# Tile 0's attention in two halves of the keys, joined by token rows

## The chip, the cores and the metric

One NeuronCore of a Trainium2 chip runs the whole program: TensorE (PE in the rows), VectorE (DVE), ScalarE (ACT), GpSimd (POOL) and the DMA queue of SyncE (SP). The metric is the device time of one execution in microseconds, the median over several runs. Lower is better.

## The reference, cut to what matters

Three steps follow each other on 12288 tokens of 128 channels: attention of q to 768 keys that are pooled from kv, and two FFNs with 2048 hidden columns.

```python
kv_pool = kv.reshape(B, H // 4, 4, W // 4, 4, C).mean(axis=(2, 4))   # 384 x 32 pixels -> 96 x 8 = 768 keys
k = v = kv_pool.reshape(B, -1, C) @ w_sr
s = (q @ k.transpose(0, 2, 1)) / np.sqrt(C)
a = np.exp(s - s.max(-1, keepdims=True))
a /= a.sum(-1, keepdims=True) + 1e-09
x = (a @ v)                                      # [12288, 128]
h = x @ w_in;   x = (h * sigmoid(1.702 * h)) @ w_out          # first FFN
h = x @ w_in2;  y = (h * clip(h + 3, 0, 6) / 6) @ w_out2      # second FFN
```

## The kernel before, in words

The tokens are cut into 24 tiles of 512. A tile has 4 slots of 128 tokens. Every fp32 product is made of three fp32r matmuls: each operand is split into a high part, copied by ScalarE (or POOL for the weights), and a low part, subtracted by VectorE (or POOL), and `product` (L799 to L802) issues high by high, high by low and low by high. Each engine has its own list of instructions, written out by hand, which it works off strictly in order; semaphores join them.

**kv and keys.** SyncE loads kv in 8 groups of 768 KB (pixels of 4 columns of the image), the last one in three rows of 256 KB, then the q tiles 0 and 1, then the four weight matrices (1 MB each), then q of tile 2. For each group VectorE adds two pairs of pixels (`add_pixels`, L566), and TensorE pools it to 96 keys with 6 matmuls against `patch` (`pool_group`, L814; a matmul of plain fp32 shows as two records). ScalarE copies the pooled part out, TensorE multiplies it by w_sr (`keys_of`, L821), ScalarE and VectorE split it into k_hi and k_lo. The values are the keys transposed by TensorE (`values_of`, L827). Keys go in parts of 384, 288 and 96; the two halves of the keys (384 each) lie in the two banks of a pair of PSUM banks.

**Tile 0 before.** Its scores (`scores`, L830 on) take all 768 keys per slot and begin once the keys' last part is split. VectorE takes the maximum (L610), ScalarE the exponential with the row sum (L406), TensorE turns the probabilities by chunks of 128 keys (`turn_probs`, L852), ScalarE and VectorE split them (L411, L632), TensorE weighs the values (`weigh_first`) into bank_av, which holds channels by tokens. 1/sum goes through DRAM to reach all partitions (`spread_inv`), and `scale_x` (L648) multiplies it in. Tile 1's scores and exponentials are slipped between these steps. `x1_high` and `x1_low` (L652) split x, ScalarE loads the table for gelu (L470), and the first FFN of tile 0 begins: `hidden1(0, p)` and `project1(0, p - 2)` for p = 0 to 7, with gelu (L438), act1_hi (L445) and act1_lo (L660) between them. The probabilities of tile 1 are transposed by VectorE (`turn_p`, L627) among these.

**Weights.** POOL splits them in 16 pieces of 512 columns (L356, L359) as they land. `hidden1(0, p)` waits for piece p // 2, `project1(0, p)` for piece 4 + p // 2, and `hidden2(0, 0)` for all of them.

**From tile 1 on** TensorE alternates jobs of the first FFN of tile i and the second FFN of tile i - 1; `between(i)` scores tile i + 2 and weighs the values of tile i + 1. This part is a loop on all engines.

Of the kernel before, what the change touches and what calls it, by code (L numbers as in the profile page):

```python
# [5 lines left out]
ALU = mybir.AluOpType  # L6
ACT = mybir.ActivationFunctionType
F32 = mybir.dt.float32
# [4 lines left out]
def attention_and_two_ffns(nc, q, kv, w_sr, w_in1, w_out1, w_in2, w_out2, out):  # L13
# [7 lines left out]
    HALF = KEYS // 2  # L21
    SLOTS = 4
# [4 lines left out]
    N_KV = KV_GROUPS * KV_ROWS * R  # L27
    GROUP_KEYS = HH // R
# [15 lines left out]
    q_rows = q.rearrange("b (n i) c -> i (b n) c", i=32)  # L44
    out_rows = out.rearrange("(n i) c -> i n c", i=32)
# [4 lines left out]
    with ExitStack() as ctx:  # L50
# [38 lines left out]
        v_hi = sb("v_hi", [128, KEYS], F32R)  # L89
        v_lo = sb("v_lo", [128, KEYS], F32R)  # L90
# [4 lines left out]
        y_sb = sb("y_sb", [128, TILE])  # L95
        w_sr_sb = sb("w_sr_sb", [128, C])
# [6 lines left out]
        p_sum_eps = sb("p_sum_eps", [128, SLOTS])  # L103
        p_inv = sb("p_inv", [128, 32])
# [5 lines left out]
        probs_first = work[:, 2 * PAIR:2 * PAIR + SLOTS * KEYS]  # L110

        pooled = p_keys[:, 0:KEYS]
        k_full = p_keys[:, KEYS:2 * KEYS]
        q_raw1, q_t1 = y_sb, x_full
        q1_hi, q1_lo = x2_hi, x2_lo

        def mid2(t, p):
# [3 lines left out]
        pair = [psum(f"pair{n}", 2 * 512) for n in range(3)]  # L121
        bank_av = psum("bank_av", 512)
        bank_out = psum("bank_out", 512)

        PART_AT = [0, HALF, KEYS - GROUP_KEYS, KEYS]
        PART_GROUPS = [KV_GROUPS // 2, KV_GROUPS - 1, KV_GROUPS]
        PART_POOL = [pair[0][:, 0:HALF], pair[0][:, 512:512 + HALF - GROUP_KEYS], bank_av[:, 0:GROUP_KEYS]]
        PART_KEYS = [pair[1][:, 0:HALF], pair[1][:, 512:512 + HALF - GROUP_KEYS],
                     bank_av[:, 128:128 + GROUP_KEYS]]
        PARTS = 3  # L130
# [7 lines left out]
        def scores_in(u, s):  # L138
            if isinstance(u, int) and u == 0:
                return pair[(0, 1, 2, 0)[s]]  # L140
            if isinstance(u, int) and u == 1:
                return pair[(1, 0, 1, 0)[s]]
            return pair[(0, 2, 1, 0)[s]]
# [8 lines left out]
        def hidden1_in(t, p):  # L152
            return pair[0] if isinstance(t, int) and t == 0 and p % 2 else pair[2]
# [16 lines left out]
        kv_row_loaded = [sem(f"kv_row_loaded{a}") for a in range(KV_ROWS)]  # L170
        q_loaded = sem("q_loaded")
        q1_loaded = sem("q1_loaded")
# [6 lines left out]
        kv_added = sem("kv_added")  # L179
# [3 lines left out]
        k_full_ready = sem("k_full_ready")  # L183
# [5 lines left out]
        qt_ready = sem("qt_ready")  # L189
# [896 lines left out]
```

## Time and profile before

| | us |
|---|---|
| median of 3 timed runs (1304.80 to 1305.52) | 1305.46 |
| the profiled execution's own time | 1302.91 |
| its span | 1301.2 |
| TensorE busy | 1275.8 (98%) |
| VectorE, ScalarE busy | 1038.3 (80%), 1031.9 (79%) |
| GpSimd busy | 38.0 (3%) |
| 16 DMA engines, queue of SyncE | 22.4% of their span |

A row of the timeline gives the start in us from the span's start, the duration (for several equal instructions in a row: from the first's start to the last's end), engine, line, operation, tiles and shapes, the count, and in brackets how long the engine had been idle and what released it. The duration of a matmul holds its way through the array; matmuls that follow each other start closer than that. The granted clock (PEclk) is a share of 2.4 GHz.

### The profile page before, as it was taken

The numbers are of one execution on the slowest core, as the hardware profiler recorded it, in microseconds if no ns is written. First come the engines' busy times: TensorE is split into PE (matmuls) and PEld (weight loads), VectorE is DVE, ScalarE is ACT, GpSimd is POOL, SyncE is SP. The second block draws the span as 40 slices with busy tenths as digits, with TensorE's granted clock in tenths as the row PEclk, the third lists the DMA queues.
The fourth block names the chain that finished last, engine by engine and source line by source line (L and its number), as shares of the span: only waits on it lengthen the run. The fifth ranks groups of instructions, "written<-read, shape, count | busy, mean of one in ns | idle before, by whom it ended". The sixth has DMA issues, their size and how long they took to land.

```text
span 1301.2 us, 18295 instructions
## 1 busy us (share of the span) xinstructions
PE 1275.8 (98%) x5748; PEld 1061.1 (82%) x5748; DVE 1038.3 (80%) x1072; ACT 1031.9 (79%) x1211; POOL 38.0 (3%) x43
## 2 busy tenths in 40 slices
PE   6899999999999999999999999999999999999998
PEld 5678888888888888888888888888888888888786
DVE  4788888878888888888788888887888888877667
ACT  2688888788888887888888878888788788887776
POOL 0910000000000000000000000000000000000000
PEclk9999999999999999999999999999999999999999
DMA  8331303213023032130230321302303213022001
GB/s 268 107 71 44 69 5 73 48 24 73 23 50 71 1 73 48 24 73 22 51 71 2 73 48 24 73 21 51 71 2 73 48 24 73 21 44 65 1 9 17
DMA packets 186884, 65.94 MB, mean 51 GB/s; under 512 B 108656, under 2 KB 179440, under 8 KB 186608
## 3 DMA queue, kind: packets, MB, share of 16 engines
q1 hardware_dynamic: 185808, 65.56, 22.4%
q10 hardware_dynamic: 1056, 0.13, 0.1%
q8 instruction: 10, 0.16, 0.1%
q14 instruction: 10, 0.08, 0.0%
HBM read 23.13 MB, written 6.34 MB: 23 GB/s over the span
## 4 chain that ended last, share of the span: by engine, by line
PE 96%; DVE 2%; ACT 1%; DMA 1%; issue 0%; SPq 0%; ACTq 0%
PE pair L800 16%; PE pair L802 16%; PE pair L801 16%; PE bank_av L800 9%; PE bank_av L802 9%; PE bank_av L801 9%; PE bank_out L802 6%; PE bank_out L801 6%; PE bank_out L800 6%; PE pair L814 1%; DMA kv_sb<-in_kv_dram 1%; DVE neg_max L610 0%; ACT probs L406 0%; DVE p_low L632 0%; DVE mid_lo L660 0%
## 5 line engine op out<-in xcount | busy, mean ns | idle before, releaser
L676 DVE TENSOR_TENSOR mid_lo<-work,mid_hi 128x1024 fp32r<-128x1024 f32 (+1 forms) x193 | 234.9, 1218 | 135.3 <-ACT mid_hi L466 135.1
L800 PE MATMUL pair<-x_hi,w_hi 128*128 128x512 f32 x768 | 301.9, 393 | 4.5 <-DVE x_lo L652 3.3
L801 PE MATMUL pair<-x_lo,w_hi 128*128 128x512 f32 x768 | 299.2, 390 | 0.0
L802 PE MATMUL pair<-x_hi,w_lo 128*128 128x512 f32 x768 | 299.0, 389 | 0.0
L438 ACT ACTIVATE work<-pair 128x1024 f32<-128x1024 f32 x192 | 197.1, 1027 | 125.0 <-PE pair L802 122.6
L660 DVE TENSOR_TENSOR mid_lo<-work,mid_hi 128x1024 fp32r<-128x1024 f32 x192 | 235.3, 1226 | 29.9 <-ACT mid_hi L445 29.9
L669 DVE SCALAR_TENSOR_TENSOR work<-work,pair 128x1024 f32<-128x1024 f32 (+1 forms) x193 | 232.3, 1204 | 4.0 <-ACT work L453 3.6
L453 ACT ACTIVATE work<-pair,half 128x1024 f32<-128x1024 f32 (+1 forms) x193 | 212.2, 1100 | 4.9 <-PE pair L802 4.9
L445 ACT ACTIVATE mid_hi<-work 128x1024 fp32r<-128x1024 f32 x192 | 202.6, 1055 | 5.1 <-PE bank_av L802 2.7
L466 ACT ACTIVATE mid_hi<-work 128x1024 fp32r<-128x1024 f32 (+1 forms) x193 | 201.4, 1044 | 1.9 <-DVE work L669 1.8
L800 PEld LDWEIGHTS pair<-x_hi,w_hi 128*128 128x128 f32 x768 | 144.1, 188 | 43.0 <-ACT work L438 7.0
L802 PEld LDWEIGHTS pair<-x_hi,w_lo 128*128 128x128 f32 x768 | 144.2, 188 | 30.5
L801 PEld LDWEIGHTS pair<-x_lo,w_hi 128*128 128x128 f32 x768 | 144.2, 188 | 28.3
L800 PE MATMUL bank_av<-mid_hi,w_hi 128*128 128x512 f32 x400 | 157.1, 393 | 1.9 <-DVE mid_lo L660 1.5
L802 PE MATMUL bank_av<-mid_hi,w_lo 128*128 128x512 f32 x400 | 155.8, 389 | 0.0
L801 PE MATMUL bank_av<-mid_lo,w_hi 128*128 128x512 f32 x400 | 155.8, 389 | 0.0
L801 PE MATMUL bank_out<-mid_lo,w_hi 128*128 128x512 f32 x368 | 143.2, 389 | 0.0
L800 PE MATMUL bank_out<-mid_hi,w_hi 128*128 128x512 f32 x368 | 143.2, 389 | 0.0
L802 PE MATMUL bank_out<-mid_hi,w_lo 128*128 128x512 f32 x368 | 143.1, 389 | 0.0
L406 ACT ACTIVATE probs<-pair,neg_max 128x768 f32<-128x768 f32 x92 | 82.5, 901 | 72.2 <-DVE neg_max L610 71.2
L610 DVE TENSOR_REDUCE neg_max<-pair 128x1 f32<-128x768 f32 x96 | 89.5, 952 | 19.9 <-PE pair L802 18.8
L800 PEld LDWEIGHTS bank_av<-mid_hi,w_hi 128*128 128x128 f32 x400 | 75.1, 188 | 23.2 <-DVE mid_lo L660 5.9
(88 smaller groups left out, 1506.9 us busy)
## 6 DMA issues: line engine op xcount, KB each, us to landing
p_keys<-p_turned SPq DMA_DIRECT2D x368, 96.0 KB, 2.2
inv_b<-inv_dram SPq DMA_DIRECT2D x24, 256.0 KB, 3.3
out_dram<-y_sb SPq DMA_DIRECT2D x94, 64.0 KB, 2.4
q_raw<-in_q_dram SPq DMA_DIRECT2D x92, 64.0 KB, 2.0
kv_sb<-in_kv_dram SPq DMA_DIRECT2D x7, 768.0 KB, 10.9
w_raw<-in_moe_w_in_dram SPq DMA_DIRECT2D x2, 1024.0 KB, 8.0
inv_dram<-inv_t SPq DMA_DIRECT2D x96, 0.5 KB
kv_sb<-in_kv_dram SPq DMA_DIRECT2D x3, 256.0 KB, 11.7
```

The costliest lines, as they stand in the source:

```text
L406: act.activation(two(slot(dst, s)), halves(scores_in(u, s)), ACT.Exp, bias=neg_max[:, s:s + 1], accum_out=p_sum[:, s:s + 1]).then_inc(exp_ ...
L438: act.activation(act1[p % 2], hidden1_in(t, p)[:, :], ACT.Gelu_apprx_sigmoid).then_inc(act1_ready, 1)
L445: act.activation(mid_hi[p % 2][:, :], act1[p % 2], ACT.Copy).then_inc(mid1_hi_ready, 1)
L453: act.activation(gate2[p % 2][:, part], hidden2_in(t, p)[:, part], ACT.Relu, bias=half[:, :], scale=1.0 / 6.0).then_inc(gate2_ready, 1)
L466: act.activation(mid_hi[mid2(t, p)][:, part], act2[p % 2][:, part], ACT.Copy).then_inc(mid2_hi_ready, 1)
L610: dve.reduce_max(neg_max[:, s:s + 1], halves(scores_in(u, s)), AX_XY, negate=True).then_inc(max_ready, 1)
L660: dve.tensor_tensor(mid_lo[p % 2][:, :], act1[p % 2], mid_hi[p % 2][:, :], ALU.subtract).then_inc(mid1_ready, 1)
L669: dve.scalar_tensor_tensor(out=act2[p % 2][:, part], in0=gate2[p % 2][:, part], scalar=1.0, in1=hidden2_in(t, p)[:, part], op0=ALU.min, op ...
L676: dve.tensor_tensor(mid_lo[mid2(t, p)][:, part], act2[p % 2][:, part], mid_hi[mid2(t, p)][:, part], ALU.subtract).then_inc(mid2_ready, 1)
L800: pe.matmul(dst, a_hi, b_hi, start=start, stop=False)
L801: pe.matmul(dst, a_hi, b_lo, start=False, stop=False)
L802: return pe.matmul(dst, a_lo, b_hi, start=False, stop=stop)
```

## The change

- kv: groups 3, 6 and 7 are loaded by rows. w_sr and q of tile 0 (token rows, 512 B each) stand behind group 1, q of tile 1 behind the last row of kv. POOL does the adds of groups 4 and 5. Keys go in parts of 288, 96, 288, 96.
- q of tiles 0 and 1 is turned by TensorE instead of VectorE. POOL splits q of tile 1, ahead of the weights.
- The values are pooled kv times w_sr, computed again in the other orientation, and v_hi and v_lo lie side by side in `v_cat`.
- Tile 0 is scored against the first 384 keys as soon as these are there, with a maximum, exponentials, a sum and an output of its own; the same follows for the second 384 keys with the maximum of both. The first half is scaled by exp(new maximum - old one) and the two are joined. The output is tokens by channels (`weigh_first`: probabilities stand, 256 columns of v_cat move), so 1/sum is a number per partition and does not go through DRAM. x is turned by TensorE.
- Tile 1's scores: slots 0 and 1 around the turning of x, slots 2 and 3 behind `hidden1(0, 0)`; its four exponentials stand behind `x1_high_first`, and the table load for gelu behind them. VectorE's four `turn_p(1, s)` and `inverse(1)` stand ahead of `act1_lo(0, 0)`.
- From tile 2 on the instructions are the same.

The lists of TensorE, ScalarE and VectorE, and the new steps that the prediction speaks of:

```diff
 # SyncE
+                if g == 1:
+                    sp.dma_start(w_sr_sb[:, :], w_sr).then_inc(w_sr_loaded, 16)
+                    sp.dma_start(q_raw[:, :].rearrange("p (s c) -> p s c", s=SLOTS), q_first).then_inc(q0_loaded, 16)
 # POOL
+            for g in POOL_GROUPS:
+                hold(kv_loaded[g], 16)
+                pool.tensor_tensor(rows[:, :, 0:2 * C], rows[:, :, 0:2 * C], rows[:, :, 2 * C:4 * C],
+                                   ALU.add).then_inc(kv_added[g], 1)
+            hold(q1_copied, 1)
+            pool.tensor_scalar(q1_hi[:, :], q_t[:, :], 1.0, 1.0, ALU.mult, ALU.mult).then_inc(q_hi_ready, 1)
+            hold(q_hi_ready, 2)
+            pool.tensor_tensor(q1_lo[:, :], q_t[:, :], q1_hi[:, :], ALU.subtract).then_inc(q_lo_ready, 1)
             for piece in range(W_PIECES):
 # VectorE, new steps
+            def maximum_first(h, s):
+                dve.wait_ge((a_scores_ready, scores_ready)[h], s + 1)
+                ...
+                dve.reduce_max(neg_max_b[:, s:s + 1], in_chunks(first_in(s)), AX_XY, negate=True).then_inc(b_max_ready, 1)
+                dve.wait_ge(a_max_ready, s + 1)
+                dve.wait_ge(b_max_ready, s + 1)
+                dve.tensor_tensor(neg_max[:, s:s + 1], neg_max_a[:, s:s + 1], neg_max_b[:, s:s + 1],
+                                  ALU.min).then_inc(max_ready, 1)
+            def join_first(s):
+                ...
+                dve.scalar_tensor_tensor(out=x_full[:, cols], in0=first_output(1, s)[:, 0:128],
+                                         scalar=scale_b[:, s:s + 1], in1=a_scaled[:, cols],
+                                         op0=ALU.mult, op1=ALU.add).then_inc(b_high_added, 1)
+                dve.wait_ge(b_high_added, s + 1)
+                dve.scalar_tensor_tensor(out=x_full[:, cols], in0=first_output(1, s)[:, 128:256], ...)
 # VectorE, its list up to the FFN
+            for g in range(KV_GROUPS // 2 - 1):
                 add_pixels(g)
+                if g == 1:
+                    q_low_first()
+            for a in range(KV_ROWS):
+                add_row_pixels(KV_GROUPS // 2 - 1, a)
             k_lo_part(0)
+            k_lo_part(1)
+            for s in range(SLOTS):
+                maximum_first(0, s)
+            v_lo_part(0)
+            p_lo_first(0, 0)
+            ...                        # row adds of groups 6 and 7, p_lo_first(0, 1..3) between them
+            k_lo_part(2); k_lo_part(3)
             for s in range(SLOTS):
+                maximum_first(1, s)
+            shift_first(); v_lo_part(1); p_lo_first(1, 0); scales_first(); a_add_low(0)
+            for s in range(1, SLOTS):
+                p_lo_first(1, s)
+            a_add_low(1)
+            for s in range(SLOTS):
+                join_first(s)
+            for h in range(2):
+                x1_low_first(h)
+            for s in range(SLOTS - 1):
+                maximum(1, s)
+            turn_p(1, 0)
+            maximum(1, SLOTS - 1)
+            for s in range(1, SLOTS):
+                turn_p(1, s)
             inverse(1)
 # ScalarE, the second half of its list
+            k_hi_copy(3)
+            q1_copy()
+            exponential_first(1, 0)
+            exponential_first(1, 1)
+            v_hi_copy(1)
+            exponential_first(1, 2)
+            p_hi_first(1, 0)
+            exponential_first(1, 3)
+            fade_first()
+            a_high_copy(0)
+            p_hi_first(1, 1); p_hi_first(1, 2); p_hi_first(1, 3)
+            a_high_copy(1)
             for s in range(SLOTS):
+                a_scale(s)
+            for h in range(2):
+                x1_high_first(h)
+            for s in range(SLOTS):
+                exponential(1, s)
             load_table(ACT.Gelu_apprx_sigmoid)
 # TensorE
+            pool_group(0); pool_group(1); turn_q_first(0); pool_group(2); pool_loaded_row(3, 0)
             pe.wait_ge(w_sr_loaded, 16)
             keys_of(0)
+            pool_loaded_row(3, 1); pool_loaded_row(3, 2); keys_of(1)
+            pe.wait_ge(k_lo_ready, 2)
+            pe.wait_ge(q_lo_ready, 1)
+            for s in range(SLOTS):
+                scores_first(0, s)
+            values_of(0); pool_group(4); turn_probs(0, 0); turn_probs(0, 1)
+            pool_group(5); turn_probs(0, 2); turn_probs(0, 3)
+            pool_loaded_row(6, 0); pool_loaded_row(6, 1); weigh_first(0, 0)
+            pool_loaded_row(6, 2); weigh_first(0, 1); pool_loaded_row(7, 0)
+            keys_of(2); pool_loaded_row(7, 1); pool_loaded_row(7, 2)
+            turn_q_first(1); keys_of(3)
             pe.wait_ge(k_lo_ready, PARTS)
+            for s in range(SLOTS):
+                scores_first(1, s)
+            values_of(1); turn_probs(1, 0); weigh_first(0, 2); turn_probs(1, 1); weigh_first(0, 3)
+            turn_probs(1, 2); pe.wait_ge(q1_copied, 1); weigh_first(1, 0); turn_probs(1, 3)
+            for s in range(1, SLOTS):
+                weigh_first(1, s)
+            pe.wait_ge(a_summed, 1)
             scores(1, 0)
+            turn_first(0); turn_first(1)
             scores(1, 1)
+            hidden1(0, 0)
+            pe.wait_ge(a_summed, 2)
+            scores(1, 2)
+            pe.wait_ge(exp_ready, SLOTS + 1)
+            scores(1, 3)
+            for p in range(1, PAIRS):
                 hidden1(0, p)
```

(Calls that stand one to a line in the code are put side by side here.)

## Rows read from the trace of the kernel before

**Rows 1.** The page, chain of waits that ended last, by engine.
```profile
PE 96%; DVE 2%; ACT 1%; DMA 1%; issue 0%; SPq 0%; ACTq 0%
```
**Rows 2.** Windows, 48 to 51 us: busy us by engine, then clock, DMA.
```profile
48.00:51.00 3.00, 0.21 (x2) 0.05 (x1) 2.64 (x6) 2.97 (x5) 2.82 (x4) 1.00 0.00 0
```
**Rows 3.** Timeline of ScalarE, 25 to 53 us.
```profile
25.05 0.25 ACT L366 ACTIVATE p_keys<-bank_av 128x96 f32<-128x96 f32 x1 [0.93 <-PE bank_av L814]
25.20 0.62 ACT L397 ACTIVATE q_hi<-q_t 128x512 fp32r<-128x512 f32 x1
...
32.35 0.90 ACT L406 ACTIVATE work<-pair,neg_max 128x768 f32<-128x768 f32 x1
...
49.57 1.28 ACT L470 ACT_TABLE_LOAD   x1
...
52.66 1.03 ACT L438 ACTIVATE work<-pair 128x1024 f32<-128x1024 f32 x1 [1.59 <-PE pair L802]
```
**Rows 4.** Timeline of TensorE, 19 to 60 us.
```profile
19.34 1.52 PE L814 MATMUL pair<-patch,kv_sb 128*128 128x96 f32 x12
...
34.39 0.34 PE L801 MATMUL pair<-k_lo,x_hi 128*128 128x384 f32 x1
34.56 0.35 PE L802 MATMUL pair<-k_hi,x_lo 128*128 128x384 f32 x1
...
35.94 1.97 PE L852 MATMUL pair<-ident,work 128*128 128x128 f32 x8 [0.49 <-ACT work L406]
...
39.34 0.60 PE L852 MATMUL pair<-ident,work 128*128 128x128 f32 x4
...
53.84 0.45 PE L800 MATMUL pair<-x_hi,w_hi 128*128 128x512 f32 x1
...
56.09 0.50 PE L800 MATMUL bank_av<-mid_hi,w_hi 128*128 128x512 f32 x1 [0.65 <-DVE mid_lo L660]
...
59.13 0.50 PE L800 MATMUL bank_av<-mid_hi,w_hi 128*128 128x512 f32 x1
```
**Rows 5.** Timeline of VectorE, the adds of kv groups and of the last row.
```profile
12.20 0.96 DVE L566 TENSOR_TENSOR kv_sb<-kv_sb 128x768 f32<-128x768 f32 x1 [1.05 <-DMA kv_sb<-in_kv_dram]
...
18.26 0.96 DVE L566 TENSOR_TENSOR kv_sb<-kv_sb 128x768 f32<-128x768 f32 x1 [1.07 <-DMA kv_sb<-in_kv_dram]
...
23.43 0.42 DVE L573 TENSOR_TENSOR kv_sb<-kv_sb 128x256 f32<-128x256 f32 x1 [0.26 <-DMA kv_sb<-in_kv_dram]
```
**Rows 6.** Windows of 1 us, TensorE alone: busy, instructions, clock, DMA share, GB/s.
```profile
12.00:13.00 1.00, 1.00 (x6) 1.00 1.02 385
...
16.00:17.00 1.00, 1.00 (x11) 1.00 1.05 385
...
36.00:37.00 1.00, 1.00 (x5) 0.50 0.95 309
```
**Rows 7.** Timeline of VectorE, 25 to 59 us.
```profile
25.85 0.69 DVE L605 SCALAR_TENSOR_TENSOR q_lo<-q_t,q_hi 128x512 fp32r<-128x512 f32 x1 [0.91 <-ACT q_hi L397]
...
27.00 0.25 DVE L580 TENSOR_TENSOR k_lo<-bank_av,k_hi 128x96 fp32r<-128x96 f32 x1
...
35.48 0.96 DVE L610 TENSOR_REDUCE neg_max<-pair 128x1 f32<-128x768 f32 x1 [0.62 <-PE pair L802]
36.36 0.18 DVE L615 TENSOR_SCALAR p_sum_eps<-p_sum 128x4 f32<-128x4 f32 x1
...
50.82 1.82 DVE L627 STREAM_TRANSPOSE p_turned<-probs 128x768 f32<-128x768 f32 x2
54.81 1.23 DVE L660 TENSOR_TENSOR mid_lo<-work,mid_hi 128x1024 fp32r<-128x1024 f32 x1 [2.17 <-ACT mid_hi L445]
...
56.84 2.23 DVE L660 TENSOR_TENSOR mid_lo<-work,mid_hi 128x1024 fp32r<-128x1024 f32 x1
```
**Rows 8.** Timeline of POOL, the first piece of the weights.
```profile
31.37 0.63 POOL L356 TENSOR_SCALAR w_hi<-w_raw 128x512 fp32r<-128x512 f32 x1 [28.73 <-DMA w_raw<-in_moe_w_in_dram]
32.18 1.27 POOL L359 TENSOR_TENSOR w_lo<-w_raw,w_hi 128x512 fp32r<-128x512 f32 x1 [0.18 <-POOL w_hi L356]
```

More of the change, by code:

```diff
@@ L109, in attention_and_two_ffns @@
         act2 = [work[:, n * PAIR:(n + 1) * PAIR] for n in (4, 5)]
[L110 to L114, printed above, removed]
+        probs_half = [work[:, at * PAIR:at * PAIR + SLOTS * HALF] for at in (4, 2)]
+        pooled = probs[:, 0:KEYS]
+        a_scaled = inv_b
+        q_raw1 = y_sb
         q1_hi, q1_lo = x2_hi, x2_lo
@@ L843, in scores, with scores_first @@
                 scores_half(u, s, 1).then_inc(scores_ready, 1)
-            def turn_probs(k):
-                if k > 1:
-                    pe.wait_ge(pt_lo_ready, k - 1)
-                else:
-                    pe.wait_ge(exp_ready, SLOTS)
-                for s in range(SLOTS):
-                    at = (k % 2) * 512 + s * 128
-                    last = pe.transpose(pair[2][:, at:at + 128],
-                                        slot(probs_first, s)[:, k * 128:(k + 1) * 128], ident[:, :])
+            def scores_first(h, s):
+                tok, keys = slice(s * 128, (s + 1) * 128), slice(h * HALF, (h + 1) * HALF)
+                if h == 1:
+                    pe.wait_ge(pt_lo_ready, s + 1)
+                product(first_in(s), q_hi[:, tok], q_lo[:, tok], k_hi[:, keys], k_lo[:, keys], True,
+                        True).then_inc((a_scores_ready, scores_ready)[h], 1)
@@ L867, in weigh, with turn_first @@
+            def turn_first(n):
+                pe.wait_ge(first_x_ready, 2 * (n + 1))
+                for c in range(2):
+                    at = (2 * n + c) * 128
+                    last = pe.transpose(X_FIRST_IN[n][:, c * 128:(c + 1) * 128], x_full[:, at:at + 128], ident[:, :])
+                last.then_inc(xt_ready, 1)
             def weigh(t, k):
@@ L887, in _ @@
+            weigh_first(0, 1)
+            pool_loaded_row(7, 0)
             keys_of(2)
-            pe.wait_ge(k_lo_ready, 1)
-            pe.wait_ge(q_lo_ready, 1)
-            scores_half(0, 0, 0)
-            scores_half(0, 1, 0)
+            pool_loaded_row(7, 1)
+            pool_loaded_row(7, 2)
+            turn_q_first(1)
+            keys_of(3)
             pe.wait_ge(k_lo_ready, PARTS)
-            scores_half(0, 0, 1).then_inc(scores_ready, 1)
+            for s in range(SLOTS):
+                scores_first(1, s)
```

509 lines of the change are left out of this document (312 added, 197 removed).

## The prediction, made before the changed kernel ran

> **What bounds the kernel now.** I read the chain of waits on the page first: TensorE holds 96% of what ended last [rows 1]. So from the second tile on, time is TensorE time, and nothing there is edited: the loop body keeps its instructions. A change to tile 0 can only move the moment at which the dense stretch begins; whatever it moves is kept to the end. Then I read windows of the first 90 us: the last large gap of TensorE ahead of tile 0's FFN is at 48 to 51 us, where it is busy for 0.21 of 3 us [rows 2]. So the event to forecast is the first gelu of tile 0: now at 52.66 us [rows 3], with the third pair of hidden matmuls at 53.84 and the first projection at 56.09 [rows 4]. Its difference is the difference of the kernels, as long as the FFN of tile 0 behind it keeps its pace.
>
> **First half, up to its scores.** VectorE adds a kv group when it lands; groups come 2.03 us apart (12.20 to 18.26 is three of them), the last row is added at 23.43 [rows 5]. Two loads (320 KB; 768 KB take 2.03 us) now stand behind group 1, so the later groups land some 0.9 us later; kv0 and kv1 land some 0.4 us earlier, w_sr no longer being ahead. By landing alone the first half's keys could be pooled at 16 us. But the queues are in order: TensorE pools group 1 (10.8 to 12.7, by 6 matmuls a microsecond, where a later one holds 11 [rows 6]), turns q with four transposes (half of eight in 1.97, 1.0 [rows 4]), ScalarE copies 0.6 [rows 3], VectorE's q_low_first takes 0.7 [rows 7] and ends at 15.1, and only behind it stand the adds of group 2 and of three rows (0.9 + 3 x 0.4). Then on TensorE: group 2 until 17.7, one row 0.5, copy 0.4, keys_of(0) 0.6, two rows 0.9, copy 0.25, keys_of(1) 0.4, k_hi and k_lo 0.25 each [rows 3, 7]. Call the start of scores_first(0, 0) A: **A = 21.3** (bounds 19.3, with TensorE at full rate and no gaps, and 23.5).
>
> **First half, from A to the second half's scores (S).** Prices: a pooling group 1.36 (12 matmuls in 1.52 with the tail of the last, 0.113 apart), a row a third of it, 0.45; a half score 3 x 0.175 = 0.52; transposes 0.088 apart (four in 0.60 with a tail of 0.25), so three 0.26 [rows 4]. weigh_first is 6 matmuls of 256 columns, a width that the trace lacks: between 0.113 (the pooling matmul, 96 columns in two passes) and 0.175 (384 columns); I take 0.122, by the line through 0.2275 at 512 and 0.175 at 384 columns, so 0.73 in all (0.68 to 1.05). TensorE's list is then: four half scores 2.1, values 0.7, groups 4 and 5 2.7, twelve transposes 1.0, rows of group 6 1.4, two weigh_first 1.5, rows of group 7 1.4, keys_of(2) 0.5, turn_q_first(1) 0.35. With the tail copy, keys_of(3), k_hi, k_lo (0.25 each with hand-overs, 1.0) it is 12.7. I walked the other engines beside it: exponential 0.58 (half of the 0.90 [rows 3] and its accumulator read), p_hi and p_lo of 384 0.5 each (between 0.25 for 96 and 0.69 for 512 [rows 7]), and they wait for TensorE more than it for them; the one tight place is pooled_copy(2) ahead of p_hi_first(0, 3) on ScalarE, which holds p_lo and the last row add until A + 10.7, just when TensorE asks for it. So **S = A + 12.7 = 34.0**. At present the same point is at 27.3 (k_lo of the last 96 keys) [rows 7]. The last kv row has then been in SBUF for about 9 us: TensorE, not the load, sets the end of this stage. POOL's adds of groups 4 and 5 (1.9 each by 1.27 for 512 elements, rows 8; at most 4) end by 21 to 25, TensorE wants group 5 at A + 4.7 = 26: covered.
>
> **Second half, from S to the FFN.** VectorE is the limit. Per slot a 384 maximum 0.5 and a one-column minimum behind its own wait 0.2 (half of 0.96, and 0.18 [rows 7]): the four maxima are out at S + 3.65. Then shift 0.2, v_lo 0.55, p_lo 0.55 (S + 5.1), four small ops behind ScalarE's fade 0.85 (S + 6.15), a_add_low 0.35, three p_lo 1.5, a_add_low 0.4 (S + 8.4), eight joins of 128 columns at 0.29 (S + 10.8). TensorE's weigh_first(1, 3) ends at S + 9.3, inside that. Turning by TensorE, x1_hi and x1_lo by halves: S + 12.0; **hidden1(0, 0) at S + 12.1 = 46.1**, where it is at 50.95 now: 4.8 us earlier. What goes with this is the trip of 1/sum through DRAM, which is no loss to anyone now (it had landed long before x_full).
>
> **But the gelu does not follow.** Before, tile 1's exponentials had been slipped between tile 0's steps and the table load lay under the wait for x1_lo. Now all four stand behind x1_high_first on ScalarE, and tile 1's slots 2 and 3 are scored behind hidden1(0, 0). From S + 12.1: hidden1(0, 0) 1.4, scores(1, 2) 1.05, scores(1, 3) 1.05 beside maximum(1, 2), then turn_p(1, 0) in VectorE's order ahead of maximum(1, 3): 15.65 + 0.9 + 0.95 = 17.5 (two turns take 1.82 [rows 7]). Exponential 1.0, table load 1.3, warm 0.25 [rows 3]: gelu at **S + 20.1 = 54.1, 1.4 us later than now**. hidden1(0, 2) waits for it until 55.2 and TensorE has nothing from 51.1 to 55.2: that gap of 4.1 us takes the place of the 2.8 us one. turn_p(1, 1..3) and inverse (3 x 0.9 + 0.6) end at S + 20.8, before act1_lo(0, 0) is due at S + 22.2: free; if they were not, each 0.9 would be added.
>
> **Behind it.** turn_p no longer interrupts act1_lo; the first projections were 3.04 apart (56.09 to 59.13) against 12 x 0.2275 = 2.73 of TensorE work [rows 4], so about -0.3. POOL waits for q1_copied and splits w from about 36.7 instead of 31.4 [rows 8]; the last piece then ends near 76 instead of 70.5, needed at about 85 by hidden2(0, 0): free. But while POOL runs, a VectorE subtract of 1024 takes up to 2.23 instead of 1.23 [rows 7], for 5 us longer: +0.3 (0 to 1).
>
> **The clock.** After 32.2 to 34.1 idle and half an us more the granted clock fell to 0.50, that is 1.2 GHz, for about 3 us, and eight transposes took 1.97 [rows 4, 6]; after the gap at 48 it stayed at 2.4 GHz [rows 2]. The new gap is longer than both. If it falls, hidden1(0, 2) costs 2.8 instead of 1.4 and project1(0, 0) begins under it: worth 1.3 by walking the first four jobs at double price until 60 us; bounds 0 and 3.3. At the front, TensorE's matmuls are slow until about 14.7 now (6 in a microsecond against 11 [rows 6]); with the added gap from 13.7 to 16 some slow rate reaches beyond A: +0.4 (0 to 2).
> The Trainium skill (TensorE: Matmul & The Clock Gate, "Why this matters for your kernels") says to leave no longer idle gaps between bursts, since the clock is halved behind them. By that rule the 1.3 us are due here; without it the sum below is 1.3 us less. It speaks against this change, and the row of 36 to 37 us agrees with it.
>
> **Sum.** +1.4 - 0.3 + 0.3 + 0.8 x 1.3 + 0.4 = about +2.8 us, with 0.8 my weight for the drop of the clock. The profiled execution's own time is 1302.91 (span 1301.2 and 1.7 around it); the timed median is 1305.46, 2.5 above it. I carry the difference over: 1305.46 + 2.6 = **1308.1 us**.
>
> **Rivals.**
> 1. The clock stays up in the new gap, and at the front: +1.4 or less, 1306.8. For it: the gap at 48 us left it alone. Against it: this one is longer, and little runs just ahead of it.
> 2. Faster. The front is set by landing and not by the order of queues: TensorE reaches the full rate before it turns q, A = 19.3 or less, and pooling overlaps so that S is near 30.5. The VectorE chain from S on has 2 us of waiting in it; with none of it gelu is at S + 18.2 = 48.7: -4.0, and 1301.6. It decides from S below 30.0 with the waits, or 31.9 without. For it: kv has landed by 23.3, and hidden1(0, 0) has 4.8 us in hand. Against it: the adds behind q_low_first, and a TensorE list of 12.7 us that is mostly price and not waiting.
> 3. Worse than forecast: scores of the first half run at 1.2 GHz, since TensorE has gaps ahead of them. The list from A gains 2 to 3 us and everything moves: +5.5 to +7, 1311.5. For it: the slow stretch at the start [rows 6]. In this case one would say that the change does not do what it says, half a tile being done "while kv loads" only on paper.
>
> **Chances.** Forecast 0.42 (own range 1306.5 to 1310.5), rival 1 0.22, rival 2 0.20, rival 3 0.16. What the measurement can tell from no change is 0.2%, 2.6 us. Faster than that is most of rival 2: 0.18. Slower is rival 3 and two thirds of the forecast: 0.44. Same: 0.38. Range 1302.0 to 1312.5: up to near rival 2, and all of rival 3 but its tail.
>
> **What would show it.** In the new trace: scores_first(0, 0) near 21.3, the last pooling matmul near 32 with kv in since 23, scores_first(1, 0) near 34, hidden1(0, 0) near 46, the gelu table load near 52.6, gelu near 54, a gap of about 4 us in TensorE before hidden1(0, 2) and a granted clock of 0.5 behind it. Wrong is the forecast if S comes before 31, if weigh_first costs over 1 us, if the exponentials of tile 1 do not hold the table load, or if the dense stretch behind tile 1's start is longer or shorter than now by over 1 us.

## The result: slower by 9.4 us, with the profile after

The kernel after takes 1314.88 us (median of 4 runs, 1314.50 to 1315.92); the kernel before, on the same chip, 1305.49 (4 runs, 1304.80 to 1306.17). By the medians that is +9.4 us (0.72%); the recorded ratio of the two kernels is a little higher, 1.0083, 95% interval 1.0071 to 1.0096. The forecast was 1308.1 (+2.6), its range ended at 1312.5: the sign was right, the size was missed by 6.8 us. The profiled execution's own time is 1315.92, its span 1314.2 (before 1302.91 and 1301.2).

Start with the chain of waits of the kernel after, by engine, beside [rows 1]:

```profile
PE 96%; DVE 2%; ACT 1%; DMA 1%; issue 0%; SPq 0%; DVEq 0%; ACTq 0%
```

Nothing new bounds the kernel. The dense stretch only starts later, and by how much is read at three places of TensorE's timeline: scores_first(0, 0), whose start the forecast calls A, scores_first(1, 0), whose start it calls S, and the first FFN, with the gap in it.

```profile
11.37 2.88 PE L996 MATMUL pair<-patch,kv_sb 128*128 128x96 f32 x12 [1.62 <-DVE kv_sb L694]
14.04 1.06 PE L1031 MATMUL bank_out<-ident,q_raw 128*128 128x128 f32 x4
17.38 2.87 PE L996 MATMUL pair<-patch,kv_sb 128*128 128x96 f32 x12 [2.28 <-DVE kv_sb L694]
20.05 1.06 PE L996 MATMUL bank_av<-patch,kv_sb 128*128 128x96 f32 x4
20.90 1.25 PE L1013 MATMUL pair<-probs,w_sr_sb 128*128 128x288 f32 x2
21.94 1.67 PE L996 MATMUL bank_av<-patch,kv_sb 128*128 128x96 f32 x8
...
25.05 0.45 PE L987 MATMUL pair<-k_hi,q_hi 128*128 128x384 f32 x1 [0.64 <-DVE k_lo L707]
25.34 0.34 PE L988 MATMUL pair<-k_lo,q_hi 128*128 128x384 f32 x1
25.51 0.33 PE L989 MATMUL pair<-k_hi,q_lo 128*128 128x384 f32 x1
...
38.04 0.45 PE L987 MATMUL pair<-k_hi,q_hi 128*128 128x384 f32 x1 [0.64 <-DVE k_lo L707]
...
45.66 0.36 PE L1076 MATMUL pair<-v_cat,p_high 128*128 128x256 f32 x1 [1.77 <-DVE p_low L804]
...
49.61 0.55 PE L1076 MATMUL pair<-v_cat,p_high 128*128 128x256 f32 x1 [2.67 <-DVE p_low L804]
49.96 0.41 PE L1077 MATMUL pair<-v_cat,p_low 128*128 128x256 f32 x1
50.17 0.41 PE L1076 MATMUL pair<-v_cat,p_high 128*128 128x256 f32 x1
...
56.90 0.50 PE L987 MATMUL pair<-x_hi,w_hi 128*128 128x512 f32 x1
...
65.94 0.77 PE L987 MATMUL pair<-x_hi,w_hi 128*128 128x512 f32 x1 [3.89 <-ACT work L548]
...
102.45 0.50 PE L987 MATMUL pair<-x_hi,w_hi 128*128 128x512 f32 x1 [1.11 <-ACT work L548]
```

A is 25.05 and S is 38.04. The rows from 20.05 to 21.94 are the three loaded rows of group 3 with keys_of(0) between them; TensorE did not wait ahead of any of them. hidden1(0, 0) is at 56.90, where it was at 50.95 before. The last row is the third pair of hidden matmuls of tile 1's FFN, the first place that looks alike in both kernels (idle 1.11 us, released by the gelu). It is called the landmark from here on; it stood at 89.42 in the kernel before. Its +13.0 us is the +13.0 us of the spans, so nothing behind it differs. (From the landmark to the end the profiles of all kernels here take 1211.8 to 1212.7 us, so a landmark tells a span to within 0.9 us.) Two waits on VectorE (1.77 and 2.67 us) stand in the middle, and behind the second the matmuls of 256 columns start 0.21 us apart (49.96, 50.17), where they start 0.12 apart elsewhere.

ScalarE's timeline answers to [rows 3]: the table load behind tile 1's last exponential, and the gelu 12.1 us later than before (64.79 against 52.66).

```profile
62.38 0.90 ACT L485 ACTIVATE probs<-pair,neg_max 128x768 f32<-128x768 f32 x1 [0.73 <-DVE neg_max L732]
...
63.38 1.28 ACT L580 ACT_TABLE_LOAD   x1
...
64.79 1.01 ACT L548 ACTIVATE work<-pair 128x1024 f32<-128x1024 f32 x1
```

Now VectorE's timeline. The first two rows are the front; then come the small operations between the maxima and the joins, and last a row of the FFN.

```profile
15.77 0.69 DVE L717 SCALAR_TENSOR_TENSOR q_lo<-bank_out,q_hi 128x512 fp32r<-128x512 f32 x1 [4.46 <-ACT q_hi L467]
...
17.24 2.71 DVE L701 TENSOR_TENSOR kv_sb<-kv_sb 128x256 f32<-128x256 f32 x3
...
39.54 0.96 DVE L744 TENSOR_TENSOR neg_max<-neg_max_a,neg_max_b 128x1 f32<-128x1 f32 x1
...
43.31 1.27 DVE L749 TENSOR_TENSOR shift<-neg_max,neg_max_a 128x4 f32<-128x4 f32 x1
...
45.44 1.19 DVE L754 TENSOR_TENSOR faded_sum<-fade,p_sum_a 128x4 f32<-128x4 f32 x1
46.67 0.54 DVE L757 SCALAR_TENSOR_TENSOR p_sum_eps<-faded_sum,p_sum 128x4 f32<-128x4 f32 x1
47.24 0.18 DVE L760 RECIPROCAL scale_b<-p_sum_eps 128x4 f32<-128x4 f32 x1
47.45 1.21 DVE L762 TENSOR_TENSOR scale_a<-fade,scale_b 128x4 f32<-128x4 f32 x1
...
65.12 0.18 DVE L790 RECIPROCAL p_inv<-p_sum_eps 128x4 f32<-128x4 f32 x1
```

The same operation on four elements takes 0.16 or 1.2 us. Put POOL's timeline beside it:

```profile
17.57 4.05 POOL L434 TENSOR_TENSOR kv_sb<-kv_sb 128x768 f32<-128x768 f32 x2 [14.94 <-DMA kv_sb<-in_kv_dram]
...
39.19 1.29 POOL L439 TENSOR_TENSOR x_lo<-q_t,x_hi 128x512 fp32r<-128x512 f32 x1 [0.18 <-POOL x_hi L437]
...
43.30 1.27 POOL L447 TENSOR_TENSOR w_lo<-w_raw,w_hi 128x512 fp32r<-128x512 f32 x1 [0.18 <-POOL w_hi L444]
...
45.33 1.28 POOL L447 TENSOR_TENSOR w_lo<-w_raw,w_hi 128x512 fp32r<-128x512 f32 x1 [0.18 <-POOL w_hi L444]
46.58 0.62 POOL L444 TENSOR_SCALAR w_hi<-w_raw 128x512 fp32r<-128x512 f32 x1
47.38 1.26 POOL L447 TENSOR_TENSOR w_lo<-w_raw,w_hi 128x512 fp32r<-128x512 f32 x1 [0.18 <-POOL w_hi L444]
...
65.03 0.61 POOL L444 TENSOR_SCALAR w_hi<-w_raw 128x512 fp32r<-128x512 f32 x1
...
69.21 2.07 POOL L447 TENSOR_TENSOR w_lo<-w_raw,w_hi 128x512 fp32r<-128x512 f32 x1 [0.19 <-POOL w_hi L444]
```

Add start and duration: the shift ends at 44.58, POOL's subtract at 44.57; faded_sum at 46.63 and 46.61; p_sum_eps at 47.21 and 47.20; scale_a at 48.66 and 48.64; the first minimum at 40.50 and 40.48. A small operation with two SBUF inputs that begins beside an instruction of POOL ends with it. The reciprocal at 47.24, with one input, falls into a pause of POOL (47.20 to 47.38) and tells nothing; the one at 65.12 runs inside POOL's w_hi (65.03 to 65.64) and still takes 0.18. It also goes the other way: POOL's subtract of 69.21, begun while VectorE's mid_lo was running (68.92 to 70.15), takes 2.07 us instead of 1.28, and VectorE's loses nothing. Taken against 0.16 each, the six that were held (the third minimum, 0.74, is not shown) cost 4.9 us, on the engine that sets the end of this stage.

The windows of TensorE alone (length, busy us with count, granted clock, DMA share, GB/s) show what its gaps bring on:

```profile
48.00:52.00 4.00, 2.39 (x11) 0.50 0.00 0
52.00:56.00 4.00, 3.69 (x21) 0.75 0.02 6
...
64.00:68.00 4.00, 2.06 (x5) 0.53 0.26 62
68.00:72.00 4.00, 4.00 (x12) 0.62 0.66 152
```

From 48 to about 54 us, and again from 66 to 71, TensorE works at 1.2 GHz.

### The profile page after: what moved, and what is told of

It reads as the page before. It is cut to its first block, busy times and chain, and to the rows that moved or that the text cites. A ratio compares the mean times of both kernels' runs of the same rounds, so it can differ in the third digit from the quotient of the medians.

```text
span 1314.2 us, 18413 instructions
## 1 busy us (share of the span) xinstructions
PE 1284.0 (98%) x5798; PEld 1071.1 (81%) x5798; DVE 1042.4 (79%) x1094; ACT 1034.9 (79%) x1228; POOL 40.5 (3%) x47
## 4 chain that ended last, share of the span: by engine, by line
PE 96%; DVE 2%; ACT 1%; DMA 1%; issue 0%; SPq 0%; DVEq 0%; ACTq 0%
PE pair L987 16%; PE pair L989 16%; PE pair L988 16%; PE bank_av L987 9%; PE bank_av L988 9%; PE bank_av L989 9%; PE bank_out L989 6%; PE bank_out L988 6%; PE bank_out L987 6%; PE pair L996 1%; DMA kv_sb<-in_kv_dram 1%; PE bank_av L996 0%; PE pair L1076 0%; PE pair L1077 0%; ACT work L563 0%
## 5 line engine op out<-in xcount | busy, mean ns | idle before, releaser
L732 DVE TENSOR_REDUCE neg_max<-pair 128x1 f32<-128x768 f32 x91 | 84.7, 953 | 18.0 <-PE pair L989 16.9
```

Source lines behind the costliest of these rows:

```text
L732: dve.reduce_max(neg_max[:, s:s + 1], halves(scores_in(u, s)), AX_XY, negate=True).then_inc(max_ready, 1)
```

## Theories

**Theory.** Four things make up the +12.1 us at the gelu, where +1.4 was forecast: A comes 3.75 us late, and three causes are put up for it (VectorE does q_low_first ahead of the adds of group 2, POOL's adds hold up the row adds, TensorE stays slow); S is 0.3 us late besides; from S to hidden1(0, 0) POOL's weight pieces hold VectorE's small operations (4.9 us), and the gap this makes in TensorE costs 1.8 us of clock (18 matmuls 0.21 instead of 0.12 us apart, and the scores behind them).

**Rivals.** The small operations are slow by themselves, behind their semaphores, whoever runs beside them. The front is set by the landing of kv. The 3.9 us gap ahead of hidden1(0, 2), and not the front, is what the change costs.

All experiments start from the kernel after, unless said otherwise. Each ratio is against the kernel before on the same chip: its median was 1304.49 us for experiments 1, 2, 4 and 5, 1304.99 for experiments 3, 6, 7 and 8, and 1306.11 for experiments 9 to 11. The kernel after was timed in its 4 runs only, on yet another occasion (before: 1305.49), so a difference to 1314.88 can be off by about 1 us. Counted against the kernel before on their own chip, the losses are 6.8 us (experiment 1), 7.1 (2), 8.9 (4), 9.5 (5) and 9.7 (6), against the 9.4 of the kernel after: the times show a gain for experiments 1 and 2, and for 5 and 6 none.

## Experiment 1: POOL starts the weights later

```diff
+            hold(scale_a_ready, 1)
             for piece in range(W_PIECES):
```

> Change: the changed kernel, but POOL begins to split the weights only when VectorE's small operations for the joining of the halves are done (it holds on scale_a_ready). Theory 1 (POOL in the way): those of VectorE's operations that read two operands from SBUF wait for POOL's tensor_tensor; then the minimum, shift, faded_sum, p_sum_eps and scale_a, now 0.54 to 1.27 us, fall to about 0.2, the stretch from the second half's scores to hidden1(0, 0) falls from 18.9 to 12.5 to 14 us, TensorE's gap of 2.7 us ahead of weigh_first(1, 1) shrinks and with it the halved clock there; the time falls by 5 to 6.5 us to about 1309. Splitting later costs nothing, since the last piece is then ready near 80 us and needed near 90. Rival: the small operations are slow by themselves, by their waits on one another; then nothing moves (within 1 us), or the time rises because hidden1(0, 0) waits for its weights. The minima beside POOL's split of q of tile 1 stay slow in both theories, 0.8 us.

Measured: 1311.32 us (6 runs, 1310.09 to 1314.74), ratio 1.0053 [1.0039, 1.0068]; 3.6 us less than the kernel after. VectorE's timeline:

```profile
39.50 0.96 DVE L745 TENSOR_TENSOR neg_max<-neg_max_a,neg_max_b 128x1 f32<-128x1 f32 x1
...
42.70 0.16 DVE L750 TENSOR_TENSOR shift<-neg_max,neg_max_a 128x4 f32<-128x4 f32 x1
...
43.92 0.16 DVE L755 TENSOR_TENSOR faded_sum<-fade,p_sum_a 128x4 f32<-128x4 f32 x1
...
44.52 0.16 DVE L763 TENSOR_TENSOR scale_a<-fade,scale_b 128x4 f32<-128x4 f32 x1
...
81.31 5.41 DVE L811 TENSOR_TENSOR p_low<-p_keys,p_high 128x1024 fp32r<-128x1024 f32 x3
```

With POOL silent the same operations take 0.16 us, and the one that still meets POOL (it splits q of tile 1 at 39.2) takes 0.96: the rival of slow small operations falls. S is the same (38.01), hidden1(0, 0) is at 51.12, S + 13.1 instead of S + 18.9, and the gap at 47 to 49.6 us is gone and with it the clock's fall (granted 1.00 there). That is 5.8 us; of these, 4.1 are the small operations, and the rest, 1.6 by the spacing of the 18 matmuls, the clock. Both went with one edit, so the clock's part is read off and not tested by itself. The last row shows where part of it goes again: POOL now splits weights until 88 us, and three subtracts of 1024 take 5.41 us instead of 3.49; TensorE waits 1.13 us at 87.37 for the x_lo that stands behind them. At the landmark -4.7 is left (97.79).

## Experiment 2: the front in another order

```diff
 # POOL, ahead of the adds of groups 4 and 5
+            hold(kv_added[KV_GROUPS // 2 - 1], KV_ROWS)
 # VectorE
                 add_pixels(g)
-                if g == 1:
-                    q_low_first()
             for a in range(KV_ROWS):
                 add_row_pixels(KV_GROUPS // 2 - 1, a)
+            q_low_first()
```

> Change: the changed kernel, but POOL adds groups 4 and 5 only after the row adds of group 3, and VectorE does q_low_first behind the adds of group 2 and 3 instead of ahead of them. Theory (order and POOL set the start A of the first half): group 2 is added as it lands, near 13.3, the three row adds take 1.2 instead of 2.7 us, A comes at 22 to 23 instead of 25.05, and the time falls by 2 to 3 us. Rival: TensorE's slow matmuls in front (about 0.24 us apart where they are later 0.12) set A; then A moves by less than 1 us and so does the time.

Measured: 1311.57 us (5 runs, 1311.43 to 1312.62), ratio 1.0053 [1.0040, 1.0066]; -3.3. TensorE's timeline:

```profile
14.32 2.71 PE L996 MATMUL pair<-patch,kv_sb 128*128 128x96 f32 x12
...
18.19 1.03 PE L996 MATMUL bank_av<-patch,kv_sb 128*128 128x96 f32 x8
...
20.65 0.45 PE L987 MATMUL pair<-k_hi,q_hi 128*128 128x384 f32 x1 [0.63 <-DVE k_lo L708]
```

A is 20.65, 4.4 us earlier, and more than was expected. The rows divide it: group 1 starts 0.57 us earlier (10.80), which is the landing of kv in this execution and not the edit; from there to group 2 it takes 2.5 us less, since TensorE has no gap between the transposes of q and group 2 (2.28 us in the kernel after); and from group 2 to A it takes 1.3 us less (6.33 against 7.67), since TensorE reaches its full rate at about 17 us (eight records in 1.03) instead of about 23 (the same eight in 1.67). In the four kernels without the gap the rate rises between 15 and 17.5 us. So the order of the queues and the slow matmuls both set A. S (33.60) follows it in full and the gelu gains 4.9 (59.93). Of that 3.6 arrives at the landmark (98.84): behind the gap of 3.89 us the clock is low for about 6.7 us here (0.50 through the whole window from 64 to 68 us), and for 5 in the kernel after.

## Experiment 3: only POOL's two kv adds later

```diff
+            hold(kv_added[KV_GROUPS // 2 - 1], KV_ROWS)      # POOL, ahead of its adds
```

> Change: the changed kernel, POOL adding groups 4 and 5 only after the row adds of group 3 (one half of front_both). Theory: the three row adds take 1.2 instead of 2.7 us and A moves from 25.05 to about 23.6; the other 3 us of front_both are the order of q_low_first and the clock that rises earlier with it. Rival: POOL has no part in it, the row adds stay at 2.7 us and A where it is.

One run: 1316.37 us, span 1314.6. VectorE's timeline:

```profile
16.77 1.09 DVE L702 TENSOR_TENSOR kv_sb<-kv_sb 128x256 f32<-128x256 f32 x3
```

The row adds take 1.09 us instead of 2.71: in the kernel after the 1.6 us between fit one of them held until the first of POOL's two adds ends (17.57 and half of 4.05 is 19.6, and the last row add ends at 19.95), though TensorE needs POOL's result only at 27.93. But the hold did not make A late: in the kernel after the last row add ends at 19.95, and TensorE comes to the first row at 20.05 and to the other two at 21.94, without a wait. A comes at 23.73 (-1.3) in this run for other reasons. Group 1 starts 0.47 us earlier (10.90), before the edit can act, and behind group 2 TensorE reaches its full rate sooner:

```profile
21.27 1.03 PE L997 MATMUL bank_av<-patch,kv_sb 128*128 128x96 f32 x8
```

Experiment 6, which leaves POOL's adds and the row adds (2.71 us) as they are, has A at 23.38. On A the rival stands: POOL has no part in it.

The gelu comes 1.6 earlier (63.15), and at the landmark 0.3 is left (102.14). The windows of TensorE:

```profile
64.00:68.00 4.00, 3.04 (x9) 0.68 0.53 123
68.00:72.00 4.00, 4.00 (x11) 0.50 0.65 148
```

Behind the same gap of 3.89 us the clock stayed low for about 7 us here (65.3 to 72.2), for 5 in the kernel after. One run does not give a time for this edit; it shows that the clock behind that gap can take back 1.3 us from one execution to the next.

## Experiment 4: tile 1's scores ahead of hidden1(0, 0)

```diff
 # TensorE
-            hidden1(0, 0)
             scores(1, 2); scores(1, 3)
+            hidden1(0, 0)
 # VectorE
-            maximum(1, 0..2); turn_p(1, 0); maximum(1, 3); turn_p(1, 1..3)
+            maximum(1, 0..3); turn_p(1, 0..3)
```

> Change: the changed kernel, but TensorE scores slots 2 and 3 of tile 1 ahead of hidden1(0, 0) and not behind it, and VectorE turns the probabilities of tile 1 only behind the fourth maximum. Theory (the exponentials of tile 1 and the table load behind them set the first gelu, not hidden1): gelu comes 1.6 us earlier after hidden1(0, 0) would have allowed it, TensorE's gap ahead of hidden1(0, 2) falls from 3.9 to about 2 us, its clock stays at 2.4 GHz behind it, and the time falls by 1.6 to 2.9 us. Rival: gelu hangs on hidden1(0, 0); then the time rises by up to 1 us.

Measured: 1313.38 us (6 runs, 1311.88 to 1317.38), ratio 1.0069 [1.0054, 1.0085]; -1.5. The gap ahead of hidden1(0, 2), at 64.42, is 1.82 us instead of 3.89, and the granted clock stays at 1.00 from 56 to 72 us. Gelu 1.5 earlier (63.27), landmark 3.1 earlier (99.38); the median of the timed runs moved by only half of that. The gap is a real cost, but the smaller one, and the rival that it is the whole price falls.

## Experiment 5: the gap filled with matmuls that nobody reads

```diff
+                if p == 2:
+                    pe.wait_ge(exp_ready, SLOTS + 3)
+                    for n in range(16):
+                        pe.matmul(bank_out[:, :], w_hi[:, 0:128], x1_hi[:, :], start=True, stop=True)
```

> Change: the changed kernel, with 16 more matmuls of 512 columns (3.6 us, their result is never read) in TensorE's gap ahead of hidden1(0, 2). Theory (the gap halves the clock for the first jobs of the FFN): the granted clock stays 1.0 from 62 to 72 us, the 8 or so matmuls that took twice the time take the usual 0.23 us, and the time falls by 0.9 to 1.3 us. Rival: ScalarE and VectorE set the pace of these jobs, the slow matmuls lie in their shadow; then the time moves by less than 0.4 us, though the clock stays up.

Measured: 1314.03 us (5 runs, 1313.47 to 1315.09), ratio 1.0071 [1.0058, 1.0084]; -0.85. The windows of TensorE:

```profile
64.00:68.00 4.00, 3.40 (x14) 1.00 0.24 58
68.00:72.00 4.00, 3.27 (x14) 1.00 0.67 152
```

This holds the gelu where it was (64.87 against 64.79) and takes away only the clock's fall. The landmark moves from 102.45 to 101.44. So the fall costs 1.0 us here, and less than five microseconds at half rate would suggest: at full rate TensorE waits 1.10 us for mid_lo at 68.73, which the slow clock had covered. The timed runs do not resolve this microsecond; it is read from the two profiles.

## Experiment 6: weigh_first(0, 0) and (0, 1) behind the second half's scores

```diff
-            weigh_first(0, 0)        # between the rows of groups 6 and 7
-            weigh_first(0, 1)
             for s in range(SLOTS):
                 scores_first(1, s)
+            weigh_first(0, 0); weigh_first(0, 1)          # two calls, around turn_probs
```

> Change: the changed kernel with weigh_first(0, 0) and (0, 1) moved behind the scores of the second half. Theory (between A and S TensorE works off a list and waits for nobody, so 1.5 us less of it is 1.5 us): S comes 1.5 us earlier and the time falls by 1 to 1.5 us, since the two products then lie in TensorE's gaps behind VectorE. Rival: VectorE or ScalarE hold S; then S moves by under 0.5 us.

Measured: 1314.67 us (5 runs, 1312.35 to 1315.99), ratio 1.0080 [1.0066, 1.0094]; -0.2, no difference. S - A falls only from 13.0 to 12.2 us, though 1.45 us of matmuls left the list: the last row add waits in VectorE's order behind p_lo_first(0, 3), and the eight records of the last rows take 1.40 us instead of 1.03. The profiled execution (1312.35, span 1310.6) is the quickest of the five; its A is early, with nothing changed ahead of it, since the half rate of the front ended for a while inside group 2:

```profile
16.89 2.04 PE L996 MATMUL pair<-patch,kv_sb 128*128 128x96 f32 x12 [2.28 <-DVE kv_sb L694]
```

Of the 1.7 us by which A is earlier here than in the kernel after, 1.2 are TensorE's rate from group 2 on, and 0.5 the earlier start. The expectation was missed: TensorE's list was not the whole price of that stage.

## Experiments 7 to 9: the edits together

combo is experiments 1, 2 and 4 in one:

> Change: the changed kernel with the edits of pool_late, front_both and scores_ahead together. Theory (the three causes add up, each lies on the one chain): A = 20.7, S = 33.6, five small operations of VectorE at 0.2 us, hidden1(0, 0) behind the scores of tile 1, first gelu at 53 us where the kernel before has 52.7; POOL ends near 78 us and still slows one or two of VectorE's subtractions; the time is 1305 to 1307, within 2 us of the kernel before. Rival: they overlap (one gap hides behind the other) and the time stays above 1308.

combo2 adds experiment 6, gives the row adds of groups 6 and 7 to POOL, and lets POOL split two weight pieces ahead of q of tile 1 and the others behind scale_a_ready:

> Change: combo, and besides: weigh_first(0, 0) and (0, 1) moved behind the scores of the second half; POOL adds the rows of groups 6 and 7 too; POOL splits two pieces of the weights ahead of q of tile 1, the rest behind scale_a_ready. Theory (TensorE's own list sets S; POOL's time before S is free): S near 32.1, first gelu near 51.6, POOL done near 74 us, and the time 1303 to 1305, a little below the kernel before. Rival: POOL's adds come later than TensorE asks for them, S does not move, and q of tile 1 waits for the two pieces; then it is no faster than combo.

combo3 is combo2 with eight unread matmuls, as in experiment 5, in the gap ahead of hidden1(0, 2):

> Change: combo2 with 8 more matmuls of 512 columns (1.8 us, never read) in TensorE's gap ahead of hidden1(0, 2). Theory (even the gap of 1.8 us lets the clock fall in some executions, by where it meets the low activity around it): the clock stays 1.0 there, the first jobs of the FFN run at full rate and the median is about 1 us below combo2, 1304 to 1304.7. Rival: with a gap this short the clock is no cost any more; then the same as combo2 within 0.4 us.

```
          median (lowest to highest)    n   ratio [95%]               A      S      hidden1(0,0)  gelu   landmark
combo     1305.51 (1304.49 - 1306.13)  11   1.0006 [0.9997, 1.0015]   19.96  32.94  49.11         52.72  90.48
combo2    1305.47 (1303.78 - 1306.87)  11   1.0007 [0.9998, 1.0016]   20.25  32.08  48.48         52.09  89.46
combo3    1304.88 (1303.58 - 1305.49)  11   0.9995 [0.9986, 1.0004]   20.31  32.13  48.54         52.15  89.51
```

The three edits of combo were worth -3.6, -3.3 and -1.5 alone; together they give -9.4 (1314.88 to 1305.51), a little more than their sum of -8.4, and the 0.5 us that are left of the loss are less than can be told. The times of the single edits are too coarse to say that they add up; the profiles say it better: at the gelu the three gain 5.8, 4.9 and 1.5 us, 12.2 in all, and combo gains 12.1. combo came out as expected. combo2 has the S that was expected (32.1) and not the time (1303 to 1305). combo3 was to be 1 us quicker than combo2 by a kept clock; the clock is kept, but from the gelu to the landmark both take 37.4 us, so the shorter fall of combo2 cost nothing there. The interval of combo3 still holds 1: no version here beats the kernel before by what can be told.

## Experiments 10 and 11: the kernel before, with POOL held back, and once more as it is

The first lets POOL of the kernel before split no weights beside the tight steps of tile 0:

```diff
             for piece in range(W_PIECES):
+                if piece == 0:
+                    hold(q_lo_ready, 2)
+                if piece == 8:
+                    hold(x1_ready, 1)
```

> Change: the kernel BEFORE (no halves), but POOL begins to split the weights only when q of tile 1 is split (q_lo_ready 2), and begins its ninth piece only when x of tile 0 is split (x1_ready 1). Theory (POOL holds up VectorE's operations with two SBUF operands, in either kernel): q_low(1) falls from 1.77 to about 0.7 us and x1_low(0) from 1.31 to 0.7, both lie on the chain that ended last, hidden1(0, 0) comes at 49.3 instead of 50.95 and the time falls by 1 to 1.7 us, to about 1303.5: quicker than both kernels. Rival: something else releases scores(1, 0) as late, or the weights come too late; then within 0.5 us of before.

Measured: 1304.72 us (11 runs, 1303.77 to 1305.37), ratio 0.9994 [0.9985, 1.0003]. VectorE's low part of q of tile 1 takes 0.68 us instead of 1.77, so POOL holds up VectorE in the kernel before too. But x1_lo still takes 1.58 (48.97), as POOL's eighth piece was not done (48.75 to 50.01), hidden1(0, 0) comes at 50.61 instead of 50.95, and the clock falls behind its gap of 3.25 us. The expected 1 to 1.7 us did not come, and the edit did not free both operations: inconclusive for the time.

> Change: none, the kernel before once more, for its profile. Its profiled execution was 2.5 us below the median of its timed runs. Theory (where TensorE's clock rises and falls differs from execution to execution, since the gaps of tile 0 are just long enough): hidden1(0, 0) again near 51 us, but the slow stretches lie elsewhere or last longer, and the time is 1304 to 1307. Rival: one profile is like the other, 1302.9, and the timed runs are longer for a reason outside of what the profile shows.

One execution of the unchanged kernel: 1306.41 us, span 1304.7, which is 3.5 us more than in the profile that the forecast rests on. The windows of TensorE of this run, beside [rows 2]:

```profile
48.00:52.00 4.00, 0.67 (x2) 0.82 0.00 0
52.00:56.00 4.00, 4.00 (x11) 0.50 0.00 0
```

The gap ahead of hidden1(0, 0) is 3.33 us here (hidden1(0, 0) at 51.50), and the clock falls behind it; in the first profile it was 2.79 and the clock stayed. The landmark is at 91.98 instead of 89.42. Of these 2.6 us, 0.55 stand already at hidden1(0, 0), so at most 2.0 are the fall's; the other 0.9 us of the 3.5 lie behind the landmark and are not explained. The profiled execution of the first profile is quicker than all timed runs beside it, so that the median of the kernel before holds such falls is likely, but was seen in one profile only.

## Why the prediction was right in its sign and wrong in its size

| step | forecast | measured | shown by |
|---|---|---|---|
| A | 21.3 (19.3 to 23.5) | 25.05 | experiment 2: 20.65 |
| S - A | 12.7 | 13.0 | the profile after |
| S to hidden1(0, 0) | 12.1 | 18.9 | experiment 1: 13.1 |
| hidden1(0, 0) to gelu | 8.0 | 7.9 | the profile after |
| gelu against before | +1.4, +1.8 with the 0.4 for the front | +12.1 | |
| from there to the landmark | +1.0 | +0.9 | |
| gap ahead of hidden1(0, 2), and the clock's fall | 4.1; 1.3, weighted 1.04 | 3.89; 1.0 | experiment 5 |

**The step that failed most is "four small ops behind ScalarE's fade 0.85", with "a one-column minimum behind its own wait 0.2" and "shift 0.2".** Their price came from a tensor_scalar with one input (0.18, [rows 7]), and they have two inputs in SBUF. The rows that warn of it were there: a subtract of 1024 takes 1.23 or 2.23 us beside POOL [rows 7], POOL's subtract lasts 1.27 [rows 8], and the forecast itself had POOL splitting weights from 36.7 us on. It charged contention only to the act1_lo behind the gelu (+0.3). The trace had a plainer warning, too: the split of q of tile 1 took 1.77 us at 32.23 where the same form took 0.69 at 25.85. What holds a large subtract for 1 us holds a tiny one for as long; eight such operations stand on the critical engine, and six of them met POOL. Measured +4.9 us, and 1.8 us more for the clock in the gap that they opened in TensorE, which had no term at all. Experiment 1 takes away 4.1 of the first and 1.6 of the second.

**A failed too, outside its bounds: the step is TensorE's rate at the front.** The place of q_low_first and the gap behind the transposes were in the forecast. What was not is that TensorE works at half rate nearly up to A. The slow stretch was said to end near 14.7 us and to cost 0.4 beyond A; it lasted to about 23. Group 1 took 2.67 us (11.37 to 14.04) where 1.9 was put, group 2 2.67 (17.38 to 20.05) where 1.7 was put, and the rest up to A 5.0 where 3.6 was put: 3.1 of the 3.75 us. The other 0.6 is that group 1 started at 11.37 and not at 10.8. Experiment 2 closes the gap, the full rate comes 6 us earlier, and A is 20.65, near the forecast's 21.3. What TensorE's rate waits for at the front stays open. The row adds took 2.71 us beside POOL where 1.2 was put; that term was wrong without effect, since TensorE came to the rows later still.

**The carrying over was wrong the other way.** The sum was made against a profile in which the clock was kept behind the gap at 48 us, and added to a median that is 2.6 us higher; experiment 11 shows one fall of the clock as a part of that. There is a slip in it besides: the terms add up to 2.8 and 2.6 was carried over. Profile to profile the loss is 13.0 us. 2.6 of it is the luck of the first profile of before (1302.91 against its median of 1305.49), 1.0 the bad luck of the profile of after (1315.92 against 1314.88); 9.4 is left.

**What held:** TensorE's list from A to S by prices (matmuls of 256 columns 0.12 us apart, as put), that TensorE and not the load sets the front's end, the gelu waiting for four exponentials and the table load, and the new gap. That the clock's fall cost near what was put is luck: behind the same gap it cost from nothing to 2.4 us, by how long the clock stayed low (last section). The trend was argued rightly: half a tile earlier is worth nothing if the gelu does not follow.

**The rivals.** Rival 1 (clock stays up, 1306.8) fell. Rival 2 (faster) asked for S below 30.0; it was 38.04, and 32.1 in the best version. Rival 3 came nearest in time (1311.5) and not in mechanism: the scores from 25.34 on start 0.17 us apart, which is the full rate. The ground it gave, the slow stretch at the start, is nevertheless what made A late.

## What to carry to other kernels

Price a small operation by who runs beside it: in every run here a VectorE instruction with two SBUF inputs ended no earlier than the POOL instruction that was running when it began, so POOL work that "is off the path" is to be placed where VectorE has no such step, or POOL is to be held back by a semaphore until the chain is through. When a stage is to be started earlier, list every consumer of its result and find the one that is late next; here it was the table load. And take the profile of before twice: two executions of one kernel lay 3.5 us apart, at most 2 of it by one fall of the clock, and the whole forecast difference was 2.6.

## What the runs showed of the hardware

- **POOL and VectorE hold each other for a whole instruction; the one that began first goes on.** A VectorE operation of 128x4 with two SBUF inputs takes 0.16 us alone, 0.54 beside a tensor_scalar of POOL, up to 1.27 beside its tensor_tensor (1.28). A larger one still does its own work behind the hold: the split of 128x512 takes 1.77 us instead of 0.69. POOL's operations are held too: 1.60 instead of 0.62 (67.42 in the kernel after), 2.07 instead of 1.28 (69.21). With one input in PSUM nothing is lost (p_low 0.54 to 0.56, the joins 0.35), nor with the reciprocal (0.18) and the transposes (0.97 for 128x768). But one input is no promise: VectorE's tensor_scalar of 128x4 takes 0.16 alone, and 0.41 in experiment 10, where it begins at 48.18 beside POOL's w_hi (47.95 to 48.57) and ends 0.02 us behind it. The Trainium skill (GPSIMD Engine Reference, "Key points") says that the two engines share their SBUF interfaces, and that VectorE's instructions collide there with POOL's when they have two SBUF inputs or run in a 2-port perf mode. By that rule, the trace agrees for the two inputs; in which mode the small tensor_scalar ran, no run here shows.
- **The length of a gap does not alone decide whether the clock falls.** It fell behind 3.89 us (the kernel after, and experiments 1, 2, 3 and 6), behind 3.33 and 3.25 (experiments 11 and 10), and behind 2.67 in six profiles; shortly ahead of that TensorE had waited 1.8 us in five of them, but only 0.76 in experiment 6. In the first profile of before it fell behind 1.78 and 0.49 (at 34.14 and 35.94). It was kept behind 2.79 (the first profile of before) and 1.82 (experiment 4, combo), and was at 0.68 in the window of a gap of 1.83 in combo2. The Trainium skill (TensorE: Matmul & The Clock Gate, "Why this matters for your kernels") warns of long idle gaps between bursts of matmuls. That warning agrees with the longer ones; between 2.67 and 2.79 the shorter gap had the fall.
- **What a fall of the clock costs depends on how long it lasts and on what is the limit behind it.** Behind the same gap of 3.89 us, the stretch from the gelu to the landmark took 36.57 us with the clock kept (experiment 5), 36.56 with it low for about 3 us (experiment 6), 37.66 with 5 (the kernel after), 38.91 and 38.99 with about 7 (experiments 2 and 3). The lost time is 0 to 2.4 us.
- **At the start TensorE works at half rate while the column of the granted clock shows 1.00:** 12 records of pooling matmuls took 2.87 us at 17.38 and 1.48 at 27.93. Where the rate rises differs from execution to execution: at about 23 us in four profiles with the gap ahead of group 2, at about 21 in experiment 3, and in experiment 6 already inside group 2 (17 us) and again after a stretch at 0.50. What holds it there is open.
